# One more row gather issued ahead of the scatters in the expert stage of an attention and mixture-of-experts kernel

## The reference

```
do_compute = x @ w_skip > 0
logits = x[do_compute] @ w_gate;  e_idx = argmax(logits);  gate_w = softmax(logits)[e_idx]
for e in range(8):
    mask = e_idx == e
    y[mask] = gate_w[mask] * (relu(xc[mask] @ w1[e]) @ w2[e])     # 512 -> 1024 -> 512
out = x;  out[do_compute] = xc + y
```

## Time and profile before

| what | us |
|---|---|
| median of 3 runs | 497.96 |
| lowest and highest of them | 495.97, 499.59 |
| the profiled execution: its time | 499.5 |
| the profiled execution: its span, from first to last instruction | 497.8 |

### The profile page before, as it was taken

The page is one execution under the profiler, slowest core; times in us unless marked ns, Lnnn a source line. Parts: engine busy times, 40 slices in busy tenths (PEclk is TensorE's granted clock), DMA queues, the critical chain, the costliest instruction groups (busy, mean ns, idle before and its releaser), DMA issues.

```text
span 497.8 us, 10511 instructions
## 1 busy us (share of the span) xinstructions
PE 460.6 (93%) x3901; PEld 344.6 (69%) x3901; DVE 221.8 (45%) x531; ACT 192.5 (39%) x407; POOL 88.0 (18%) x136
## 2 busy tenths in 40 slices
PE   8799997777998979879999999999999999999995
PEld 7678775643444434568888888888888888888884
DVE  5677775622132222435555564443314544333332
ACT  8565653001222212414555545343324434333332
POOL 6856551030434434300000000000000000000000
PEclk9999997799999999989999999999999999999999
DMA  8999985879977089092000000200000002000002
GB/s 225 250 322 326 285 313 188 313 279 393 394 250 281 24 321 375 17 369 95 0 3 0 21 22 0 93 35 0 0 9 33 0 0 84 0 0 0 0 0 84
DMA packets 30626, 67.27 MB, mean 135 GB/s; under 512 B 3400, under 2 KB 9552, under 8 KB 30592
## 3 DMA queue, kind: packets, MB, share of 16 engines
q1 hardware_dynamic: 28960, 64.49, 38.0%
q0 software_dynamic: 1344, 1.76, 1.1%
q10 hardware_dynamic: 288, 0.52, 0.3%
HBM read 60.03 MB, written 7.73 MB: 136 GB/s over the span
## 4 chain that ended last, share of the span: by engine, by line
PE 56%; DMA 1%; DVE 0%; issue 0%; ACT 0%; DVEq 0%; POOLq 0%; SPq 0%
PE bank L1382 9%; PE bank L1384 9%; PE bank L1383 9%; PE bank L1363 9%; PE bank L1361 9%; PE bank L1362 9%; PE bank L1345 1%; DMA xrow<-x_rows 1%; PE bank L1063 1%; DMA x_rows<-y_out,sidx 0%; DVE x_sb L1022 0%; DVE stage L1033 0%; ACT x_sb L710 0%; DVEq L322 0%; POOLq L322 0%
## 5 line engine op out<-in xcount | busy, mean ns | idle before, releaser
L1382 PE MATMUL bank<-w_r,ghi 128*128 128x512 f32 x192 | 76.7, 399 | 0.0
L1383 PE MATMUL bank<-w_r,ghi 128*128 128x512 f32 x192 | 75.9, 395 | 0.0
L1384 PE MATMUL bank<-w_r,glo 128*128 128x512 f32 x192 | 75.9, 395 | 0.0
L1361 PE MATMUL bank<-x_sb,w_r 128*128 (+1 forms) x192 | 75.2, 392 | 0.7 <-DVE x_sb L1022 0.7
L1363 PE MATMUL bank<-x_sb,w_r 128*128 (+1 forms) x192 | 75.8, 395 | 0.0
L1362 PE MATMUL bank<-x_sb,w_r 128*128 (+1 forms) x192 | 75.1, 391 | 0.0
L1042 DVE TENSOR_TENSOR act_g<-act_g,clipped 128x512 f32<-128x512 f32 x48 | 33.3, 693 | 77.3 <-ACT clipped L728 77.3
L727 ACT ACTIVATE act_g<-bank,minus_c 128x512 f32<-128x512 f32 x48 | 33.0, 688 | 87.1 <-DVE clipped L1040 87.1
L1044 DVE TENSOR_TENSOR glo<-act_g,ghi 128x512 fp32r<-128x512 f32 x48 | 33.2, 693 | 34.8 <-ACT ghi L731 34.8
L731 ACT ACTIVATE ghi<-act_g 128x512 fp32r<-128x512 f32 x48 | 30.3, 632 | 37.7 <-DVE act_g L1042 22.8
L1040 DVE TENSOR_SCALAR clipped<-bank 128x512 f32<-128x512 f32 x48 | 33.0, 687 | 26.6 <-PE bank L1363 26.6
(11 more groups left out here) (172 smaller groups left out, 570.2 us busy)
## 6 DMA issues: line engine op xcount, KB each, us to landing
w_f<-w SPq DMA_DIRECT2D x64, 512.0 KB
v_sb<-vW SPq DMA_DIRECT2D x8, 585.0 KB, 6.8
w_f<-w_in SPq DMA_DIRECT2D x8, 512.0 KB, 7.9
w_f<-w_out SPq DMA_DIRECT2D x8, 512.0 KB, 9.3
k_raw<-kT SPq DMA_DIRECT2D x8, 400.0 KB, 6.7
q_sb<-qT SPq DMA_DIRECT2D x16, 192.0 KB, 8.9
x_rows<-x_pair SPq DMA_DIRECT2D x8, 384.0 KB, 5.6
out<-stage SPq DMA_DIRECT2D x12, 256.0 KB, 2.2
```

The costliest lines, as they stand in the source:

```text
L1361: mm(bank[f % 2][:, :], hi, x_hi, start=(c == 0), stop=False)
L1382: mm(bank[4 + i][:, :], hi, w_hi, start=(f == 0), stop=False)
L1383: mm(bank[4 + i][:, :], hi, w_lo, start=False, stop=False)
L1384: last = mm(bank[4 + i][:, :], lo, w_hi, start=False, stop=(f == F2C - 1))
```

## The change

The order in which GpSimd issues gathers and scatters. Six gathers stand ahead of the first scatter in place of five; then a scatter and a gather take turns as before, but the gather that follows S(n) is G(n+6), of the same parity, in place of G(n+5). The number of gathers (20), of scatters (18) and of rounds of the loop stays, and nothing changes on other engines.

```diff
             for parity in range(2):
                 pool.wait_ge(x_stored[parity], 16 * PAIRS // 2)
-            for par in (0, 1, 0, 1, 0):
+            for par in (0, 1, 0, 1, 0, 1):
                 gather(par)
-            scatter(0)
-            gather(1)
             pool.wait_ge(counts_done, 1)
             half = half_tiles(pool)
             with pool.Fori(0, half - 2) as i:
-                for par in (1, 0):
+                for par in range(2):
                     scatter(par)
-                    gather(1 - par)
-            for par in (1, 0, 1):
+                    gather(par)
+            for par in (0, 1, 0, 1):
                 scatter(par)
```

## The result

| | before | after |
|---|---|---|
| median, first comparison, us | 497.3 (4 runs) | 490.2 (4 runs, 489.07 to 490.89) |
| ratio after to before | | 0.9857, 95% interval 0.9822 to 0.9893 |
| ratio in a second comparison, more runs | | 0.9827, 95% interval 0.9761 to 0.9894 |
| the profiled execution: time, span, us | 499.5, 497.8 | 489.85, 488.1 |

Some executions of either kernel are over 1.5% longer than its fastest, and all ratios here leave them out. The changed kernel is 7.1 us faster, 1.4%.

A forecast was written before the change was run, and what follows sets the result against it. TensorE was taken to bound the kernel, stalled by late gathers. 499.5 less 5.1 (stage) and 0.4 (tail) gave 494.0 us; the middle between that and a median of 492.5 gave 493.3, range 490.6 to 497.0.

The forecast's parts named there:

- The bound and the stall: Expert stage: TensorE, 93% busy, loses 5.5 us waiting for `xs`, as gathers queue behind scatters; all should go.
- G(5) and the pairs: GpSimd's list: G(5) at about 117.6, 8.5 us earlier; later gathers 1.3 us behind a scatter, about 4.9 us earlier.
- Covered under load: G(16), moved into the load, needs 7.3 us and has 7.5 until VectorE, about 2 more until TensorE.
- What is late next: only TensorE's own rate: Expert stage without stalls: 4.875 us a tile by `h_sb`, 68.25 us for 14 tiles, giving back 5.1 us.
- Rival A: Expert stage: TensorE runs at 4.56 us a tile once nothing stalls it; 488.9 us, chance 0.10.
- The tail: Behind tile 17's `h_sb`, 7.8 us to the last scatter: shorter by 0 to 0.7 us, taken as 0.4.
- The median: Profiled execution 1.5 us above the median: excess lies elsewhere, giving 492.5, or in stalls, giving 494.0; middle 493.3.
- C: Expert stage: TensorE's waits stay, as earlier gathers meet the weight transfers at another place; 498.0 us, chance 0.08.
- D: Expert stage: results wait for scatters landing later than 8.85 us, against landings up to 8.0; 503.5 us, chance 0.04.
- The figure of 2.15 us: Estimated time for a 64 KB gather from GpSimd; by it G(15) is in time and the change worth nothing.

The follow-up runs named there:

- 1: Kernel before, with weight loads of experts 5 to 7 and the first eight dense-stage pieces cut to an eighth: 488.85 us, ratio 0.9847.
- 4: Kernel before, with only the weights of expert 7 and the first eight dense-stage pieces cut to an eighth: 492.55 us.
- 6: Against the kernel before: gathers held until the old moment but issued ahead of the scatter, 1.3 us earlier: 489.87 us.
- 9: Changed kernel with GpSimd memsets: three between scatter and gather, 489.2 us; six ahead of both, 494.34 us and 493.97 in the repeat.
- 3: Kernel before, unchanged, profiled twice more: 500.19 and 494.94 us.
- 5: Changed kernel, unchanged, profiled twice more: 489.23 and 493.01 us.
- 2: Changed kernel, with weight loads of experts 5 to 7 and the first eight dense-stage pieces cut to an eighth: 488.19 us, ratio 0.9833.
- gather-first kernel: Changed kernel with each loop pair swapped, gather ahead of scatter: ratio to the kernel before 0.9831, then 0.9885 in more rounds.

## Why the prediction was off

- **The bound and the stall.** Right. TensorE limited the stage, its 5.5 us of waits for `xs` came from gathers queued behind a scatter, and a cut of the traffic (1, 4) or an earlier issue (6, the change) removes them.
- **G(5) and the pairs.** Right. G(5) is at 117.15 (117.6 in the prediction), gathers stand 1.3 us behind the scatter, G(15) at 166.33 is 10.1 us earlier and in the quiet stretch as foreseen, and no wait is added.
- **Covered under load.** Right. TensorE never waits for `xs` after tile 2; G(16), in the load, had 6.9 us until VectorE turned to it where the prediction had 7.5, and that was enough. The run with the gather 1.5 us later shows that there is room left.
- **"What is late next: only TensorE's own rate", 4.875 us a tile.** This step failed. I took it from `h_sb` on VectorE in tiles 9 to 13 of one execution. Three profiles of the changed kernel give 4.58 to 4.59 (64.3, 64.1, 64.1 us for 14 tiles), the fourth, with the lag, 4.64; two more of the kernel before give 4.57 in their quiet tiles, and so does the quiet run of its order. The prediction took a rate that held in one execution for that of the kernel. These 14 tiles gave back 73.35 - 64.3 = 9.1 us in the profiled executions, not 5.1, and against the other two profiles of the kernel before the whole stage gave back 7.4 to 7.9, where the forecast had 5.5 with its tail.
- **Rival A.** This was the right case, and I gave it 0.10; 4.6 us a tile was the prediction's own sign for it. Its rate, 4.56 by the starts of `up` in the earlier trace rows, is what the runs show. Its time, 488.9, is 1.3 us too low, probably because it too was reckoned from an execution whose stage of 84.2 us was longer than the 82.7 and 83.2 of the other two.
- **How I chose.** The prediction set 4.875, the mean of four tiles on VectorE, against 4.56, a single tile on TensorE, and called them the same tiles. Over the same four, tiles 9 to 13, the starts of `up` in the kernel before give 174.41 - 155.65 = 18.76 us, 4.69 each, since tile 12 took 4.98:

```profile
155.65 1.93 PE L1274 MATMUL bank<-w_f,xT 128*32 128x256 f32 x32
...
174.41 1.93 PE L1274 MATMUL bank<-w_f,xT 128*32 128x256 f32 x32
```

  The Trainium skill, "Perfetto Trace Analysis", section "Tensor Engine Instruction", says that TensorE's end times are estimated, but it has the starts as reported times, and 4.56 was a difference of starts. The rule gave no ground against it. Neither row could settle the matter alone: the lag was in this execution, and only further profiles showed that it was no property of the kernel.
- **The tail.** I added 0 to 0.7 us of shortening. It rested on the lag as a steady state and has no ground: in the changed kernel `h_sb` to the last scatter takes 199.39 - 190.42 = 9.0 us, longer than the 7.8 before.
- **The median.** The profiled execution of before lies 2.2 us above the median of 497.3, that of after 0.35 below its own, so 9.65 us between them are 7.1 between the medians. The prediction asked whether such an excess lies elsewhere or in long stalls; some 2 us of lag were a third possibility. How much of the 2.2 is lag isn't shown, since what lies outside the stage differs by 5.7 us between the three profiles of before. The median of before also came out 0.7 us lower with a fourth run (497.3 for 497.96), which is 0.7 of the 3.1 us by which the forecast missed.
- **Rivals C and D.** C fell. D did not occur, but the kernel with late pairs in 9 shows that the place was real: a landing of 6.9 us, one stall of 2.7 to 3.3 us. D's price was read from the wrong transfers. In that trace the line of the earlier trace rows holds no gather and no scatter, as the profile has no landing for them there; its 8.0 is of a 256 KB load of the dense stage. Where the profiles give the landings of scatters, the longest is 6.2 us in the kernel before and 6.4 in the changed one (profiles of 3 and 5). In the changed kernel a scatter has 172.86 - 165.01 = 7.9 us from its start, of S(9), until `result`, of tile 11, wants it landed, so 1.5 us were to spare, and the 8.85 of the prediction was about 1 us too many.
- **The figure of 2.15 us** for a gather, from "DMA: Bandwidth & Descriptors" of the Trainium skill, section "Anatomy of one DMA": this is near the shortest landings in these profiles, 2.3 us (third profile of the kernel before), and under load the measured ones are 5.5 us and more. That the kernel before lost its time to the loaded gathers is what 1 and 2 show.

**Open.** What makes VectorE and ScalarE start 3 us and more behind `up`. It was there at length in two profiles of seventeen, one of either order, and in seven tiles of the second one of the gather-first kernel; in the two it costs some 2 us. In nearly all of its tiles in these two, `h_sb` starts 0.6 to 0.8 us behind the end of an indirect DMA's issue on GpSimd. In the quiet tiles of the other executions of these two kernels it starts while such an issue still runs (126.16 in the kernel after, with the gather from 125.36 to 126.39), so it doesn't always wait for the end of one. Whether the one depends on the other isn't shown, and no run here puts it to the test. Open is also the 1.2 us and more at one `down` near the end of the stage, seen in two profiles of the kernel before, in that of 6 and in the second one of the gather-first kernel.

## What to carry to other kernels

Where one in-order list issues both the fetches for later work and the stores of finished work, put each fetch as far ahead as its buffer allows. Being late costs next to nothing while there is slack, and then more with each step: 1.5 us later than in the changed kernel cost at most 0.5 us, 3.3 us later 2.6 us (over 1 of it in the `down` that is open above), one tile later 7 to 9 us and two tiles later 53. The stores have a limit of their own: pushed behind the fetches, they were waited for in turn.

Before a rate is taken from one execution, compare two engines' rows over the same stretch, all of it and not one tile. Where they disagree, something in that execution isn't steady, and a second profile of the same kernel says more than a choice between the rows.

## What the runs showed of the hardware

A 64 KB gather from HBM landed after 2.3 us at the least, 5.5 us in the median and 6.5 at the most in the third profile of the kernel before; with most of the traffic gone (1) the median was 3.2. In the first profile rows were copied 2.9 us after the gather's start at a DMA share of 0.08, and 7.3 us after it at 0.99. A scatter of the same size landed after 2.3 us in the median with most of the traffic gone (2) and after 5.3 in the second profile of the changed kernel, and in 9 one was waited for until 6.9 us after its start.

The issue of such a gather or scatter keeps GpSimd for 1.0 us, with 0.3 us between two in a row.

Stalls of 2.99 us (first profile), 2.25 us (4) and 2.66 us (9) were each followed by a granted clock of 0.61 to 0.68 over some 4 us. One of 1.6 us in the second profile of the kernel before and one of 3.27 us in the repeat of 9 were followed by 1.00. So the length of the stall alone doesn't tell.

Five waits of 5.4 us in all cost 6.2 us of stage at a granted clock of 1.00.
